# Attention and two matrix networks in one kernel: token chunks of 384 instead of 256, attention units of three tiles in two PSUM banks, block means by vector sums

## The reference, cut to what matters

```python
# attention: q, k, v of (2 batches, 8 heads, 768 rows, 64); blocks of 32 keys
k_sum = k.reshape(B, H, nb, 32, D).max(axis=3)
v_sum = v.reshape(B, H, nb, 32, D).mean(axis=3)
scores_l = where(|i - j| < 16, scale * q @ k.T, -1e9)
scores_s = scale * q @ k_sum.T + log(32)
a = softmax(concat([scores_l, scores_s]))
x = a @ concat([v, v_sum])                # to (1536 tokens, 512)
# first network: 512 -> 2048 -> 512
y = relu(x @ w_in) ** 2 @ w_out
# second network: 512 -> 1024 -> 512
h = y @ w2_in
solu = h * softmax(h)
out = (layer_norm(solu) * g) @ w2_out
```

## Time and profile before

| | |
|---|---|
| three runs, us | 515.67, 513.10, 515.68; median 515.67 |
| the profiled execution, us | 513.74, of which its span 512.0 |
| PE busy | 490.3 us, 96% of the span |
| DVE, ACT, POOL busy | 250.7, 219.5, 45.6 us |
| moved by DMA | 39.38 MB |

### The profile page before, as it was taken

One profiled execution on the slowest core, in us unless ns is written; L12 is line 12 of the kernel. 1 busy time (PEld: TensorE's weight loads), 2 busy tenths in 40 slices (PEclk: granted clock), 3 DMA queues, 4 the chain that ended last, 5 costly groups with the idle time before them and its releaser, 6 DMA issues.

```text
span 512.0 us, 9826 instructions
## 1 busy us (share of the span) xinstructions
PE 490.3 (96%) x3936; PEld 451.0 (88%) x3936; DVE 250.7 (49%) x504; ACT 219.5 (43%) x573; POOL 45.6 (9%) x65
## 2 busy tenths in 40 slices
PE   2678999999999999999999999999999999999997
PEld 2458999999999999999999999999988888888885
DVE  3438878744445434544345433456764444444340
ACT  2357677444343343544445432344443333333331
POOL 1123445100000200000000000000000000000000
PEclk9989999999999999999999999999999999999999
DMA  8484763231102100030002002223221221000011
GB/s 274 164 252 126 203 214 114 72 135 57 58 27 89 38 24 25 17 109 27 27 27 84 1 1 83 84 83 96 77 76 61 70 84 34 20 22 20 22 41 41
DMA packets 26397, 39.38 MB, mean 77 GB/s; under 512 B 1824, under 2 KB 13216, under 8 KB 26352
## 3 DMA queue, kind: packets, MB, share of 16 engines
q1 hardware_dynamic: 26352, 38.76, 23.4%
HBM read 31.41 MB, written 7.34 MB: 76 GB/s over the span
## 4 chain that ended last, share of the span: by engine, by line
PE 91%; DVE 5%; issue 1%; ACT 1%; DMA 1%; POOL 0%; DVEq 0%; ACTq 0%
PE bank L760 26%; PE bank L735 26%; PE bank L855 12%; PE bank L828 12%; PE bank L681 5%; PE bank L694 3%; PE bank L724 3%; PE bank L709 3%; PE bank L843 2%; DVE probs L526 1%; DVE neg_max L530 1%; DMA k_raw<-kT 1%; ACT probs L384 1%; DVE probs L541 1%; DVE solu L643 1%
## 5 line engine op out<-in xcount | busy, mean ns | idle before, releaser
L735 PE MATMUL bank<-x_hi,win_hi 128*128 128x256 f32 x384 | 110.6, 288 | 0.7 <-POOL win_lo L347 0.7
L760 PE MATMUL bank<-h_hi,wout_hi 128*128 128x256 f32 x384 | 109.2, 284 | 0.2
L760 PE MATMUL bank<-h_lo,wout_hi 128*128 128x256 f32 x384 | 108.6, 283 | 0.0
L760 PE MATMUL bank<-h_hi,wout_lo 128*128 128x256 f32 x384 | 108.6, 283 | 0.0
L735 PE MATMUL bank<-x_hi,win_lo 128*128 128x256 f32 x384 | 108.5, 283 | 0.0
L735 PE MATMUL bank<-x_lo,win_hi 128*128 128x256 f32 x384 | 108.5, 283 | 0.0
L553 DVE TENSOR_TENSOR sqr<-relu 128x256 f32<-128x256 f32 x96 | 44.5, 464 | 102.0 <-ACT relu L426 102.0
L426 ACT ACTIVATE relu<-bank 128x256 f32<-128x256 f32 x96 | 36.6, 381 | 103.6 <-PE bank L735 102.4
L735 PEld LDWEIGHTS bank<-x_hi,win_hi 128*128 128x128 f32 x384 | 73.5, 191 | 1.6 <-POOL win_lo L347 1.2
L760 PEld LDWEIGHTS bank<-h_hi,wout_hi 128*128 128x128 f32 x384 | 73.6, 192 | 1.4 <-issue 1.3
L760 PEld LDWEIGHTS bank<-h_lo,wout_hi 128*128 128x128 f32 x384 | 73.7, 192 | 0.0
(11 more groups left out here) (69 smaller groups left out, 700.4 us busy)
## 6 DMA issues: line engine op xcount, KB each, us to landing
v_ext<-vwin SPq DMA_DIRECT2D x24, 188.0 KB
win_raw<-w_in_t SPq DMA_DIRECT2D x8, 512.0 KB, 13.8
wout_raw<-w_out_t SPq DMA_DIRECT2D x8, 512.0 KB, 13.0
win_raw<-w_t SPq DMA_DIRECT2D x8, 512.0 KB, 3.5
k_raw<-kT SPq DMA_DIRECT2D x8, 399.0 KB, 6.3
q_sb<-qT SPq DMA_DIRECT2D x24, 128.0 KB, 3.8
out<-o_sb SPq DMA_DIRECT2D x12, 256.0 KB, 2.0
y_dram<-x_hi SPq DMA_DIRECT2D x4, 512.0 KB, 3.1
```

Of the source, the lines that this page charges most:

```text
L735: last = nc.tensor.matmul(up_bank(n), win[a][:, f * WC + k * P:f * WC + (k + 1) * P], x[b][:, c % 2, k * CH:(k + 1) * CH], start=(k == 0 a ...
L760: last = nc.tensor.matmul(down_bank(d), wout[a][:, f * WC + d * P:f * WC + (d + 1) * P], h[b][:, n % 3, :], start=(f == 0 and a == 0 and b ...
```

## The change

- `CH` is 384, so there are four chunks and 64 steps of 24 matmuls with 384 moving columns.
- A unit has three tiles (192 tokens). There are 32 units, eight for each chunk (`UPC`), and units 0 to 7 come before the loop. After that a slot comes every second step, and in the first chunk at steps 0, 2, 4, 5, 7, 9, 10, 12 and 13. A slot's order is `values`, `turned`, `scores`.
- The four `down` accumulators now take banks 2 to 5 whole, so that from unit 8 on attention has banks 0 and 1: scores and the third transposed tile in bank 0, two transposed tiles and the values in bank 1. `copy_probsT` is split: the last third (`copy_last`) waits for `maxima` of the next unit, and `x_high` for the transposes of the next unit. Units 0 to 7 still alternate between two sets of banks.
- The second batch's block means are `tensor_reduce` sums on DVE, from four loads of v in another layout, one multiplication, and four small transfers into `v_ext`.
- y is split and saved in quarters. The loads of the start are reordered.

```diff
-CH = 256
+CH = 384
+TPU = 3
+UPC = HPC * PPB
-SLOTS = {0: (None, 4, 5), 4: (4, 5, 6), 7: (5, 6, 7), 10: (6, 7, 8), 13: (7, 8, 9)}
-for _u in range(8, UNITS):
-    SLOTS[4 * (_u - 4)] = (_u, _u + 1 if _u + 1 < UNITS else None, _u + 2 if _u + 2 < UNITS else None)
+SLOTS = {0: (None, 8, 9), 2: (8, 9, 10), 4: (9, 10, 11), 5: (10, 11, 12), 7: (11, 12, 13), 9: (12, 13, 14),
+         10: (13, 14, 15), 12: (14, 15, 16), 13: (15, 16, 17)}
+for _u in range(2 * UPC, UNITS):
+    SLOTS[2 * (_u - UPC)] = (_u, _u + 1 if _u + 1 < UNITS else None, _u + 2 if _u + 2 < UNITS else None)
+V_AT = {6: 0, 8: 1, 10: 2, 12: 3}
...
         def scores_bank(u):
-            return bank[:, 0 if u % 2 == 0 else 3, 0:UC]
+            return bank[:, 2 * (u % 2) if u < UPC else 0, 0:UC]
+        def turned_bank(u, t):
+            if u < UPC:
+                return bank[0:KX, 1 + 2 * (u % 2), t * P:(t + 1) * P]
+            return bank[0:KX, 1, t * P:(t + 1) * P] if t < TPU - 1 else bank[0:KX, 0, UC:UC + P]
         def down_bank(d):
-            return bank[:, 4 + d // 2, (d % 2) * CH:(d % 2 + 1) * CH]
+            return bank[:, 2 + d, 0:CH]
...
+            def copy_last(u):
+                act.wait_ge(masked_ok, min(u + 2, UNITS))
+                nc.scalar.copy(probsT[0:KX, u % 2, 2 * P:3 * P], turned_bank(u, 2)).then_inc(probsT_ok, 1)
             def x_high(u):
                 act.wait_ge(attn_ps, u + 1)
+                if u >= UPC:
+                    act.wait_ge(probsT_ps, min(u + 2, UNITS))
+                if u >= 2 * UPC:
+                    act.wait_ge(y_saved[u % PPB], 32 * (u // UPC - 1))
...
          def _(act):
...
             for n in range(STEPS):
...
+                if n in SLOTS and SLOTS[n][1] is not None:
+                    copy_last(SLOTS[n][1])
-                if n - 1 in SLOTS and SLOTS[n - 1][2] is not None:
-                    exps(SLOTS[n - 1][2])
                 if n + 2 < STEPS:
                     hidden(n + 2)
+                if n in SLOTS and SLOTS[n][2] is not None:
+                    exps(SLOTS[n][2])
...
          def _(pool):
...
+            windows_k(UPC)
             w_in_low(2)
             w_in_low(3)
+            windows_k(UPC + 1)
...
         def _(sp):
...
+            for p in range(PPB):
+                sp.wait_ge(attn_ps, p + 1)
+                load_vw(PPB + p)
             load_w(wout_raw, w_out_t, 0, wout_in)
             load_w(win_raw, w_in_t, 1, win_in)
...
+            def sums_v(j):
+                dve.wait_ge(vn_in, 16 * (j + 1))
+                nc.vector.tensor_reduce(v_sum[:, j * VD:(j + 1) * VD],
+                                        v_next[:, :].rearrange("p (d b) -> p d b", b=BLOCK), AX.X, ALU.add)\
+                  .then_inc(vsum_ok, 1)
...
         def _(pe):
...
                     if a is not None:
                         values(a)
+                    if b is not None:
+                        turned(b)
                     if c is not None:
                         scores(c)
-                    if b is not None:
-                        turned(b)
                 up(n + 2)
-                if n in MEAN_AT:
-                    means(1, MEAN_AT[n])
                 down(n)
```

More of the change, by code:

```diff
@@ L46 @@
 LAST = (NCHUNK - 1) * F1
+VP = 4
+VD = P // VP
 SK = S // P
@@ L258, in _ @@
[L258 to L268, removed]
+            for p in range(PPB):
+                if p >= 2:
+                    sp.wait_ge(scores_ok, PPB + p + 1)
+                    load_q(UPC + p)
+                sp.wait_ge(attn_ps, PPB + p + 1)
+                load_vw(UPC + p)
@@ L269, in _ @@
+            for g in range(3, F1 // WG):
                 load_w(win_raw, w_in_t, g, win_in)
                 load_w(wout_raw, w_out_t, g - 1, wout_in)
+                if g == 5:
+                    load_vn(0)
             load_w(wout_raw, w_out_t, F1 // WG - 1, wout_in)
[L272 to L277, removed]
+            for u in range(UPC, UNITS):
+                if u >= 2 * UPC and u % UPC == 0:
+                    save_y(u // UPC - 2)
@@ L305, in _ @@
             sp.wait_ge(xlo_ok, UNITS)
-            for c in range(2):
-                sp.wait_ge(y_saved[c], 32)
+            for d in range(KD):
+                sp.wait_ge(y_saved[d], 32)
             load_y(0)
@@ L311, in _ @@
                 load_w2(g)
-            for c in range(2):
-                sp.wait_ge(y_saved[c], 64)
+            for d in range(KD):
+                sp.wait_ge(y_saved[d], 64)
             for i in range(TT + 2):
@@ L353, in _ @@
                 summaries_k(0, p)
-            windows_k(4)
+            for u in range(PPB, UPC):
+                windows_k(u)
             w_in_low(0)
             w_in_low(1)
-            windows_k(5)
+            windows_k(UPC)
             w_in_low(2)
             w_in_low(3)
+            windows_k(UPC + 1)
             for n in range(LAST):
@@ L767, in _ @@
             scores(1)
+            means(0)
+            scores(2)
             turned(0)
-            scores(2)
             turned(1)
-            means(0, 0)
+            values(0)
             scores(3)
-            values(0)
+            means(1)
+            scores(4)
+            means(2)
+            values(1)
             turned(2)
-            means(0, 1)
-            values(1)
-            means(0, 2)
+            scores(5)
             values(2)
             turned(3)
-            means(0, 3)
-            up(0, range(0, 2))
+            means(3)
+            scores(6)
+            turned(4)
             values(3)
-            scores(4)
+            scores(7)
+            turned(5)
+            values(4)
+            values(5)
+            up(0, range(0, 1))
+            turned(6)
+            up(0, range(1, 2))
+            values(6)
+            turned(7)
+            scores(8)
+            up(1, range(0, 2))
+            values(7)
             up(0, range(2, 3))
-            up(1, range(0, 3))
+            up(1, range(2, 3))
             up(0, range(3, 4))
@@ L827, in _ @@
                             for a, b in PASSES:
-                                last = nc.tensor.matmul(bank[:, 2 * p + half, :], y_tile(s, a, k),
+                                last = nc.tensor.matmul(bank[:, (0, 6)[p] + half, :], y_tile(s, a, k),
                                                         w2[b][:, (k * FH + half) * WC:(k * FH + half + 1) * WC],
@@ L842, in _ @@
                     for f in range(F2):
-                        last = nc.tensor.transpose(bank[:, 6 + f // 4, (f % 4) * P:(f % 4 + 1) * P],
+                        last = nc.tensor.transpose(bank[:, 2 + f // 4, (f % 4) * P:(f % 4 + 1) * P],
                                                    cen[:, 1 - p, f * P:(f + 1) * P], ident[:, 0:P])
```

337 lines of the change are left out of this document (202 added, 135 removed).

## The result

| | before | after |
|---|---|---|
| median of the runs | 514.75 us (513.10 to 515.68, 4 runs) | **527.21 us** (525.79 to 529.10, 4 runs) |
| ratio to before, with its 95% interval | | 1.0248 [1.0202, 1.0294] |
| span of the profiled execution | 512.0 us | 525.3 us |

What follows compares the result with a forecast made beforehand. PE's issue was taken to bound the loop, and a chain over PE, DVE and ACT the start. Start +3.9, loop -18.9 and second network +1.3 gave -13.7, span 498.3 and 501 us, range 496 to 506.

Steps and rivals of the forecast that it cites:

- its load ... issued at 31 it lands at 34.5: Start: the first w_out load, behind `load_vw(7)`, takes 3.5 us; ACT stands at `w_out_high(0)` until it lands.
- the start: Everything before the loop's `up(2)`: eight units of three tiles move it from 44.59 to 48.5, +3.9 us, bounds 0 to +18.
- the spreads go out after `values(15)` at step 13 ... Zero on the path.: Loop, second batch's means: SP's small spreads have 12 us before step 16 needs them, adding nothing.
- Three waits of 0.9, 2.7 us.: Touching slots at steps 4-5, 9-10, 12-13: PE waits for softmax behind relu and square; bounds none or 2 us each.
- Three quarters of 0.62 + 0.96 + 0.41 is 1.49, plus the fixed 0.16: 1.65.: Loop slots: values, scores and transposes shrink with tiles from four to three; 22 full slots make 36.3 us.
- 384 columns at 173.3 ns: Loop matmuls: 160.0 ns of columns plus a 13.3 ns surcharge whatever the width; 1488 matmuls take 257.9 us.
- rival 3: Fewer, wider matmuls save nothing, the surcharge belonging to columns: 180 ns each, 10 us back, 511 us; chance 0.04.
- the second network +1.3: Behind the loop: the last two `down` steps have 24 matmuls at 173.3 ns instead of 120, adding 1.3 us.
- Earlier isn't possible: Lower bound of the start, +0: first scores still wait for POOL at 5.16 and every engine has more to do.
- Rival 1: The start keeps the old pace because latency rules: +16 to +18 us, near 511 to 513; chance 0.17 including halfway, 507.
- Rival 2: The start's units run one behind another: `values(7)` at 70, 29 us more, 530 us; chance 0.05.
- Rival 4: Attention chain holds PE in every slot through shared bank 0: 11 us over 22 slots, 512 us, or less, 506; chance 0.10.

Runs made afterwards that it cites:

- e1: The changed kernel with the v windows loaded as 96 rows (two rows of zeros added) instead of 94: 515.22 us.
- e9: e7 with the v windows back at 94 rows: 508.43 us.
- e5: The changed kernel with v windows as 96 rows, `load_vn` ahead of `load_k` on SP, and POOL's `windows_k` ahead of `w_in_low`: 502.85 us.
- e6: e5 with the first w_out load moved right behind the first w_in load: 499.02 us.
- e7: e6 with a slot's softmax (exps and normalise) ahead of the hidden layer on ACT and DVE: 495.51 us.
- e10: e5 without moving `load_vn` ahead of `load_k`, so the changed kernel with 96 rows and POOL's windows first: 502.71 us.
- e4: The kernel before the change, with transposes ahead of scores inside a slot and all else as it was: 518.44 us.
- e8: The kernel before the change, with the v windows loaded as 96 rows: 513.84 us.

## Why the prediction was wrong

- **"its load ... issued at 31 it lands at 34.5 if it takes the 3.5 us of an undisturbed weight load, not the 13.0 of a loaded queue."** This step failed, and with it the largest term, the start, by 12.3 us. I took the undisturbed price and never asked what loaded the queue in before. The 13.0 in the earlier trace rows was the warning. The load was issued at 34.73 and took 9.56, so w_out came 9.8 us late: 6.1 by the load itself, 3.7 by its issue. The late issue is a load too, one for which the prediction has no term: the second part of the mask took 11.2 us and held DVE for 8.73, and `values(3)` came at 33.51 instead of about 30. With 96 rows what was laid by hand for the start holds within 2 us: `values(5)` at 30.4 (forecast 32), w_out usable at 33.1 (34.5), `values(7)` at 41.7 (41), `up(2)` at 49.23 (48.5). So the start is wrong by its loads alone (e1), and not by w_out in particular: in e9 the mask and q pay the same price. The change made them visible: eight units instead of four need their windows in the start, and half the mask is loaded among them. The Trainium skill, "DMA: Bandwidth & Descriptors", section "Why a DMA increments its semaphore by 16 and not by 1", says that a transfer issued from SP uses the largest number of engines, 16 at most, that divides the slowest dimension of both its sides. That makes 2 for 94 rows and 16 for 96. The traces agree: shares of 0.12 and 0.13, about 2 of 16, while only 94-row windows were under way, and 0.73 with 96 rows. I hadn't weighed this page.
- **"the spreads go out after `values(15)` at step 13 ... Zero on the path."** For the spreads it held. But the loads of the same means stand on SP behind a wait for POOL, and the prediction named only DVE's 5 us. DVE stood 4.2 us.
- **"Three waits of 0.9, 2.7 us."** For what it described, the softmax behind the hidden layer, it measured 0.66 + 0.66 + 1.35 = 2.7 (e5), and turning the order gave 2.9 (e6 to e7). That the sum fits to a tenth is luck: no single wait was 0.9, and the prediction's own marks, 5.5 less 4.7, give 0.8. Missing were POOL's windows behind `w_in_low` at the same slots. For the loop's entry the prediction follows just this order, with 1.5 us of POOL in the chain to `up(2)`; it didn't ask the same of steps 5 and 10. Mending the order gave 8.9 us in the loop and 3.0 at the entry (e5, e10), more than the 4.5 us of waits in the loop that the timelines of e1 and e5 name as gone, since in e1 part of PE's work behind them ran at the lower clock (`up(2)` 4.01 us, the `up` of step 10 3.48, instead of 2.08).
- **"Three quarters of 0.62 + 0.96 + 0.41 is 1.49, plus the fixed 0.16: 1.65."** Measured 1.94, 6.4 us over 22 slots. I scaled by tiles and missed that the order within the slot changes too; by e4 that is 0.2 of the 0.29. The other 0.1 fits parts of a group that don't shrink with its tiles: `values` 0.50 and `scores` 0.75 instead of 0.465 and 0.72. That part was argued, not tested.
- **Clock.** The sum has no term for it. In the changed kernel PE idles in the start and again at steps 9 and 10, the granted clock is 0.72 on average from 36.75 to 60 us, and `up(2)` takes 4.01 us for 2.08. Each long wait thus cost more than its length.
- **What held.** 384 columns at 173.3 ns, against rival 3; the second network +1.3; no block means on PE in the loop; y by quarters with no wait; a loop of 302.5 in e7 against a forecast of 299.9, although each slot there still costs 1.94: 22 times 0.29 is 6.4 more, and the 2.7 of touching slots and about 1 us of small waits are gone.
- **"Earlier isn't possible"**, the lower bound of the start, doesn't hold either. The first scores of e7 still start at 5.14, but `up(2)` comes at 41.06, 3.5 us earlier than in before, with eight units ahead of it: the idle time of PE took them in, and more.
- **The rivals.** Rival 1 priced the start as it came out, +16, but by latency, and e1 shows that latency wasn't it. Rival 2 would have shown `values(7)` past 58; it came at 53.25, and at 41.7 in e1. Rival 4 fell: in slots that don't touch, PE shows no wait. What none of them had was transfers in the start, together with a queue's order in the loop.

With 96 rows and POOL's order mended, and nothing else, the kernel takes 502.7 us (e10), near the forecast of 501. That is in part a coincidence: the dearer slots (+6.4) are partly made up for by an earlier `up(2)` (46.7 against 48.5), and by 1.4 us of waits of the old loop that the forecast had kept. The spans are 3.6 apart, 501.9 against 498.3; the times are only 1.7 apart because the forecast adds 2.7 to its span, and e10's median lies 0.8 above the span profiled.

## What to carry to other kernels

When a change needs more loads in the start, look at each one's row count and at its landing time in the trace, and ask why a landing takes four times that of the same load elsewhere; this is worth an edit of its own even if, as in e8, it gains nothing yet. For every slot that is moved closer to its neighbour, follow all queues to it, SP's and POOL's too, and ask what stands in each ahead of the item that PE needs. If one late item is mended and the time hardly moves, look for what had made it late rather than for the next waiter.

## What the runs showed of the hardware

- The same v windows, as 94 rows (141 KB) or 96 (144 KB): with nothing but narrow ones moving the DMA share is 0.12 to 0.13 at 44 to 50 GB/s; as 96 rows one moves, with a q load, at 0.73 and 211 GB/s. The loads among them are slowed as well: the w_out loads of 512 KB land in 12.5 us instead of 8.6 (medians), the first one in 9.56 instead of some 4.4, and in e9 one q load of 96 KB takes 9.1.
- Four transposes of 128 columns take 0.41 us ahead of full-height matmuls and 0.58 ahead of matmuls on 64-row tiles (before and e4).
- The granted clock followed PE's idle stretches closely. Windows of the changed kernel:

```profile
47.00:52.00 5.00, 4.91 (x34) 3.72 (x34) 2.04 (x7) 1.68 (x6) 0.00 (x0) 0.50 0.26 87
52.00:56.00 4.00, 4.00 (x30) 3.48 (x30) 1.53 (x4) 2.14 (x9) 1.22 (x1) 0.99 0.28 96
56.00:60.00 4.00, 1.26 (x10) 0.92 (x11) 3.90 (x7) 2.93 (x7) 2.03 (x3) 0.86 1.05 312
60.00:65.00 5.00, 5.00 (x23) 4.70 (x20) 1.91 (x4) 0.27 (x1) 0.00 (x0) 0.50 1.06 349
```

  Behind the wait of 7.93 us PE works at 0.50 (1.2 GHz) from 47 to 52 us and at 0.99 (2.4 GHz) from 52 to 56; behind a stretch in which it was busy for 1.26 of 4 us it is again at 0.50, and `up(2)` falls into that: its matmuls start every 320 ns (61.27, then 61.59) instead of 173. In e7, where PE is busy for 22.45 of the 23.25 us up to 60, the clock is 1.00 throughout.
